# Hidden rows turned in 32 by 32 squares by VectorE and moved by DMA, for every other block of the first network

## What is computed

```python
# attention: state = alpha * state + k v^T; y = q . state      -> x (3072, 384)
expert_idx = np.argmax(xn @ en.T / tau, axis=1)                # 8 experts
for e in range(8):
    mask = expert_idx == e
    h = np.maximum(x[mask] @ w1[e], 0.0)                       # 384 -> 1024
    out[mask] = gate_w[mask, None] * (h @ w2[e])               # 1024 -> 384
h = out @ w_in                                                 # 384 -> 2048
y = np.maximum(0.01 * h, h) @ w_out                            # 2048 -> 384
```

## Time and profile before

| | us |
|---|---|
| median of 3 runs | 841.24 |
| lowest, highest | 840.91, 841.72 |
| the profiled execution's own time | 841.14 |
| its span, first to last instruction | 839.4 |
| PE busy | 826.0 |
| DVE busy | 418.4 |
| ACT busy | 340.4 |

### The profile page before, as it was taken

How to read it: one execution, slowest core, us unless ns; L and a number is a source line. 1 busy time by engine, 2 the same in 40 slices (tenths; PEclk the granted TensorE clock), 3 DMA queues, 4 the chain that set the end, 5 groups by cost and what they waited for, 6 DMA issues and landing times.

```text
span 839.4 us, 16998 instructions
## 1 busy us (share of the span) xinstructions
PE 826.0 (98%) x5491; PEld 742.7 (88%) x5492; DVE 418.4 (50%) x652; ACT 340.4 (41%) x643; POOL 197.4 (24%) x280
## 2 busy tenths in 40 slices
PE   7899999999999999999999999999999999999998
PEld 7788887999999999999999998998998998998997
DVE  7899986735544435445265433533533433443332
ACT  2545554634544425445254323323323333333223
POOL 6667623132233222332124003003003001000100
DMA  9988664435345332496002201201101000000001
GB/s 227 273 248 238 195 217 136 165 108 188 112 130 189 104 115 104 129 241 201 26 4 41 38 1 39 38 1 38 21 17 38 0 0 36 3 1 3 36 1 38
DMA packets 50454, 78.44 MB, mean 93 GB/s; under 512 B 22695, under 2 KB 39635, under 8 KB 50416
## 3 DMA queue, kind: packets, MB, share of 16 engines
q1 hardware_dynamic: 41232, 63.05, 26.1%
q0 software_dynamic: 5888, 14.85, 5.2%
q10 hardware_dynamic: 3296, 0.06, 0.2%
HBM read 63.69 MB, written 15.64 MB: 95 GB/s over the span
## 4 chain that ended last, share of the span: by engine, by line
PE 93%; DMA 3%; DVE 2%; POOL 1%; issue 1%; ACT 0%; SPq 0%; POOLq 0%; DVEq 0%
PE bank L1471 24%; PE bank L1506 24%; PE bank L1444 15%; PE bank L1424 15%; PE bank L1435 3%; DMA qkas<-qka 2%; PE bank L1266 2%; PE bank L1306 2%; PE bank L1283 2%; PE bank L1314 1%; PE bank L1400 1%; PE bank L1272 1%; PE bank L1326 1%; POOL kt L560 1%; DVE decay L874 0%
## 5 line engine op out<-in xcount | busy, mean ns | idle before, releaser
L1471 PE MATMUL bank<-yT,wts 128*128 128x512 f32 x864 | 217.0, 395 | 0.0
L1506 PE MATMUL bank<-wts,gs 128*128 128x384 f32 x1152 | 215.4, 335 | 0.4 <-ACT os L823 0.2
L1506 PEld LDWEIGHTS bank<-wts,gs 128*128 128x128 f32 x1152 | 202.1, 188 | 10.6 <-issue 1.6
L1471 PEld LDWEIGHTS bank<-yT,wts 128*128 128x128 f32 x864 | 160.7, 188 | 30.7
L1232 DVE TENSOR_TENSOR g<-bank,small 128x512 f32<-128x512 f32 x96 | 66.4, 692 | 174.1 <-ACT small L832 167.0
L1424 PE MATMUL bank<-wts,gxT 128*128 (+1 forms) x549 | 139.5, 398 | 0.2 <-issue 0.2
L1444 PE MATMUL bank<-wts,hT 128*128 x744 | 137.2, 339 | 0.0
L832 ACT ACTIVATE small<-bank 128x512 f32<-128x512 f32 x96 | 57.6, 600 | 187.3 <-PE bank L1471 165.7
L1444 PEld LDWEIGHTS bank<-wts,hT 128*128 128x128 f32 x744 | 128.5, 188 | 0.2
L1424 PEld LDWEIGHTS bank<-wts,gxT 128*128 128x128 f32 x549 | 100.2, 188 | 19.3 <-issue 0.8
L1234 DVE TENSOR_TENSOR gs<-g,gs 128x512 fp32r<-128x512 f32 x96 | 66.6, 693 | 67.0 <-ACT gs L835 61.5
(11 more groups left out here) (178 smaller groups left out, 728.9 us busy)
## 6 DMA issues: line engine op xcount, KB each, us to landing
raw<-w SPq DMA_DIRECT2D x14, 1536.0 KB, 7.2
qkas<-qka SPq DMA_DIRECT2D x20, 675.5 KB, 5.4
vs<-v SPq DMA_DIRECT2D x24, 192.0 KB, 3.8
x_rows<-xs SPq DMA_DIRECT2D x24, 192.0 KB, 3.9
yl<-y_rows SPq DMA_DIRECT2D x20, 192.0 KB
raw<-w_in SPq DMA_DIRECT2D x2, 1536.0 KB, 7.0
raw<-w_out SPq DMA_DIRECT2D x2, 1536.0 KB, 7.7
raw<-w SPq DMA_DIRECT2D x3, 512.0 KB, 5.5
```

The costliest lines, as they stand in the source:

```text
L1471: m = pe.matmul(gps[f % 2][:, :], wts[:, 0, w_part, n:n + P], yT[:, u, y_part, k], start=(k == 0 and (w_part, y_part) == (0, 0)), stop=(k ...
L1506: m = pe.matmul(ops[tt], gs[:, f % 4, g_part, tt * P:(tt + 1) * P], wts[:, 1, w_part, f * D:(f + 1) * D], start=(f == 0 and (g_part, w_par ...
```

## The change

For the even blocks 2, 4, ..., 28 (14 of the 31; `by_squares`), PE no longer turns the hidden rows. ACT writes ReLU's result to `hr`; DVE turns every 32 by 32 square of it within its 32 partitions (`turn_h` on DVE, one `transpose` of 128 by 512 for each half) into `hs`; SP issues 16 transfers of 32 partitions by 256 numbers (`move_h`, 1 KB rows) that bring the squares to their partitions in `hds`; ACT and DVE make `hT` from `hds`, in SBUF, in place of the banks. The rows of `w2` are put in another order ahead of the launch, so that the order of the hidden columns fits; ReLU of the other blocks writes its columns in that order too.

PE is two blocks ahead with `w1`: in the step of block `w` it does `hidden(w + 2)`. In the steps of odd blocks `turn_h(w)` stands between the halves as before, in those of even blocks nothing does. POOL gathers one block further ahead. Weights: the split of the next expert's `w1` is made two blocks ahead, in the step `w` where `w + 2` is an expert's first block, that of `w2` where `w` is. ACT makes the splits and then itself waits for DVE's part (`w1_lo`, `w2_lo`) and issues the load of the half after (`load_half`), 16 loads; SP keeps the first two. `wtab`'s flags are fewer, so DVE makes seven small vectors less before the first step. All weights come from one array in which a partition's 12 KB lie together (2 KB pieces; 4 KB and 1.5 KB before). Both first tiles of the second network's inner product stand before the last `contract`.

```diff
+        def by_squares(w, u):
+            return u == 0 and not (isinstance(w, int) and w in (0, WINDOWS - 1))
...
+        def load_half(eng, half, n):
+            eng.wait_ge(w_lo[half], n * 3)
+            at = slice(half * 3 * PC, (half + 1) * 3 * PC)
+            src = weights[n, half] if isinstance(n, int) else weights[ds(n, 1), half].rearrange("a p n -> (a p) n")
+            eng.dma_start(raw[:, at], src, max_dma_last_dim=2048).then_inc(raw_in[half], 16)
...
 SP
+            def move_h(w):
+                for j in range(QUADS):
+                    if j % 2 == 0:
+                        sp.wait_ge(h_turned, w - FIRST + j // 2 + 1)
+                    if j == 0 and not (isinstance(w, int) and w == FIRST):
+                        sp.wait_ge(ht_lo, w * 2 - 2)
+                    for i in range(QUADS):
+                        sp.dma_start(hds[j * SQ:(j + 1) * SQ, i * QF:(i + 1) * QF],
+                                     hs[i * SQ:(i + 1) * SQ, 0, j * QF:(j + 1) * QF]).then_inc(h_moved, 16)
...
 ACT
+            def h_round(w, u, half):
+                cols = slice(half * HALF, (half + 1) * HALF)
+                if not by_squares(w, u):
+                    act.wait_ge(ht_turned, turns_by_pe(w) + half + 1)
+                    act.activation(hT[:, 0, cols], htps[half][:, :], ACT.Copy).then_inc(ht_hi, 1)
+                    return
+                act.wait_ge(h_moved, w * 128)
+                act.wait_ge(ye_ready, w + 1)
+                act.activation(by_square(hT[:, 0, cols]), moved(half), ACT.Copy).then_inc(ht_hi, 1)
+            def first_weights(s, e):
+                wait_from(act, h_ready, s * 2)
+                split_hi(act, e, next_set(act, e), W1_PIECES)
+                load_half(act, 0, next_expert(act, e))
+            def second_weights(w, e):
+                act.wait_ge(ye_ready, w + 1)
+                split_hi(act, e, next_set(act, e), W2_PIECES)
+                load_half(act, 1, next_expert(act, e))
...
+            def step(w, u):
+                if isinstance(w, int) and w == 0:
+                    for half in range(2):
+                        relu(1, 1, half)
...
                 for half in range(2):
+                    h_round(w, u, half)
+                if isinstance(w, int) and w == 0:
+                    gx_round(2, 0)
+                    with act.If(act.snap(E - first) > 0):
+                        first_weights(0, 1)
+                if ahead(w, 2):
+                    for half in range(2):
+                        relu(w + 2, u, half)
+                if ahead(w, 3):
+                    gx_round(w + 3, 1 - u)
+                if ahead(w, 2):
+                    e, first = follower(act, w + 2)
+                    with act.If(first > 0):
+                        first_weights(w + 2, e)
+                e, first = follower(act, w)
+                with act.If(first > 0):
+                    second_weights(w, e)
...
 DVE
+            def turn_h(w, u):
                 for half in range(2):
+                    dve.wait_ge(relu_done, w * 2 + half + 1)
+                    dve.transpose(hs[:, u, half * HALF:(half + 1) * HALF].rearrange("p (n f) -> p n f", f=SQ),
+                                  hr[:, half].rearrange("p (n f) -> p n f", f=SQ)).then_inc(h_turned, 1)
...
+                for half in range(2):
+                    h_rest(w, u, half)
...
+                if ahead(w, 2) and by_squares(w + 2, u):
+                    turn_h(w + 2, u)
+                if ahead(w, 3):
+                    gx_rest(w + 3, 1 - u)
                 if isinstance(w, int) and w == 0:
                     place_slots()
...
 PE
+            def step(w, u):
+                if isinstance(w, int) and w == 0:
+                    block_hidden(1, 1)
+                if isinstance(w, int) and w == 0:
+                    turn_h(0, 0)
+                    turn_gx(2, 0)
+                if ahead(w, 2):
+                    block_hidden(w + 2, u, (lambda: turn_h(w, u)) if u == 1 else None)
+                elif not by_squares(w, u):
+                    turn_h(w, u)
+                if ahead(w, 3):
+                    turn_gx(w + 3, 1 - u)
+                if not ahead(w, 1):
+                    pe.wait_ge(w_lo[0], SET_IN * 3 + 3)
+                    pe.wait_ge(relu_done, WINDOWS * 2)
+                    for f in range(2):
+                        inner(0, 0, f)
...
                 contract(w, u, par)
```

More of the change, by code:

```diff
@@ L987, in _ @@
             W = WINDOWS
[L988 removed]
+            expert, first, code = (wflag[:, j, :] for j in range(3))
             start("side", dve.memset(cx, 0.0))
[L990 removed]
             start("side", dve.memset(first, 1.0))
```

276 lines of the change are left out of this document (132 added, 144 removed).

## The result

The changed kernel takes **846.6 us** in the median of 6 runs (843.48 to 847.44); the kernel before took 841.22 in its 6 (840.91 to 841.87). The ratio is 1.0054, 95% interval 1.0035 to 1.0074: slower by half a per cent, where 837.3 was forecast. The profiled execution took 847.34, its span is 845.3, 5.9 more than before's 839.4.

What follows compares the result with a forecast made beforehand. PE, busy 98% of the span, was taken to bound the kernel. From 841.14, -11.1 and -0.3, then +2.8, +1.4, +1.5 and +1.8 gave 837.2, or 837.3 on the median's scale; range 832.5 to 841.8.

Steps and rivals of the forecast that it cites:

- Removed transposes: PE's list in 14 even blocks: eight transposes of 0.79 us go from each, -11.1 us in all.
- The bound from above: Removed transposes: half 1's 0.08 longer time goes too if it came from the transposes ahead, -12.2 us.
- What replaces them in the loop: DVE's turning, SP's 16 moves and the rounding in even blocks: hidden by some 6 us of cover, cost 0.
- Weights on ACT: ACT's splits, wait for DVE and issue of loads: 0.9 us of cover left in the tightest odd step, cost 0.
- Step 0: `hidden(2)` stands right behind `turn_gx(2)`, whose result it reads: a PE gap of 2.8 us, bounds 1.4 and 4.
- step 29: `h(29)` is turned and contracted with nothing between: PE waits 1.5 us, bounds 1.1 and 1.6.
- The end: The third tile waits for `g` of the first, no longer covered by the second tile: +1.8 us, bounds 0 and 2.1.
- Earlier tables: Seven DVE vectors go before the first step, so `hidden(1)` may start at once: -0.3 us, bounds -0.4 and 0.
- Step 1: PE waits for `hT(1)` behind ACT's and DVE's splits and tables: a gap of 1.4 us, bounds 0 and 3.
- The rival of the slower clock: PE at half clock for another 5.06 us behind the gap in step 0: 2.5 us more, 839.8; chance 0.09.
- The rival of lost cover: Splits' steps or DVE's longer list overrun their cover in the loop, 0.3 us a block over 14: 841.4; chance 0.07.
- The other rivals: Moves set the pace, 910, chance 0.07; the gaps are not there, 831.8, 0.10; half 1 slower, 846, 0.03.

Runs made afterwards that it cites:

- the fills: The changed kernel with 12 fill matmuls of PE in the wait of step 0 and 11 in that of step 1: 842.21 us.
- the run with late loads: The changed kernel with ACT issuing each load of weights one step later, between the two ReLUs of the next block: 843.19 us.
- Four orders: Changed kernel, 846.6; its start and end in the old order, 843.38; ACT and DVE reordered in steps 0 and 1, 845.25; all four edits, PE turning block 2, 837.03.
- the last of the four orders: The changed kernel with one table read, other start order, both end edits, and PE turning block 2 too (`FIRST` 4): 837.03 us.

## Why the prediction was wrong

*Removed transposes, -11.1.* Mis-sized, in the good direction: -13.3. An even block lost 0.90 and the odd one behind it 0.05. The bound from above, -12.2, was too tight. I took the 0.79 between two starts as the whole price, but half 1 behind the transposes also ran 0.08 longer (2.16 against 2.08), and the rest, 0.03 and 0.05, I had nowhere.

*What replaces them in the loop, 0.* Right in the end, on wrong numbers, so with luck. An issue took 0.591 us, not 0.43, so 16 took 9.4 to 9.6; still under the 0.96 at which I had it decide. Sixteen fixed costs of 2 us one behind the other would be 32 us a pair, and the pair took 18.15, so they do overlap; the Trainium skill (DMA: Bandwidth & Descriptors, Anatomy of one DMA) gives those 2 us for transfers that GpSimd issues, and these are SP's. But the cover was not 6 us: beside a load of weights the rows landed so late that ACT waited 4.91 for them, and `hT` was ready 0.85 before PE wanted it (253.56 + 1.29 against 255.70). In eight of the even blocks ACT waited so for moved rows, 5.1 us on average, and in blocks 10 to 18 between 0.5 and 1.2 was left. I had put both on separate queues and taken them as apart.

*Weights on ACT, 0.* **This is the step that failed.** It put the cover behind a split in an odd step at 0.9 and the cost at nothing; it cost 5.5. For the splits of `w1` I had the time at which ACT is free right, 11.9 into the step (214.93 is 12.0 in). I then let ACT round at once. It did not: 1.38 us of register work lie between, and rounding, rest and PE's start took 1.72 where I had 1.28. For the splits of `w2` ACT was free only at 12.9 (235.25), since both reads stood ahead of the split, with 0.54 behind. Either way cover 0.9 became a wait of 0.8 to 1.0 and its restart, four times: +4.8; block 3 the same way, +0.7. The sum had no term for register work on ACT at all.

How much of it is the read that the change added (ACT and DVE read twice a step where they read once)? From `contract(2)` to `contract(30)` the kernel gains 2.3 us when ACT reads once and 2.5 when DVE does too. So the added read is nearly half of the 5.5. The rest stays with one read: four waits of 0.42 to 0.48 with their restarts, in steps where ACT also waits for DVE's last piece and issues. Its parts were not told apart. By the Trainium skill (Advanced Engine Details and Errata, Control Flow Timing) a branch with a compare takes about 0.1 us; the trace's rows of ACT's branch behind a read have 0.034 to 0.050, a small part of a read's 0.68, of which the load takes 0.285.

*Step 0, +2.8*: 2.88, and *step 29, +1.5*: 1.27 and the restart, 1.5. *The end, +1.8*: 1.62, 1.9 with the restart. *Earlier tables, -0.3*: -0.24, and `hidden(1)` did follow at once. *Step 1, +1.4*: 2.48, within its bounds of 0 to 3. ACT's chain there had the same hole, and DVE, too, idled 2.05 us behind `place_slots`.

*The rival of the slower clock* (0.09, +2.5) came true as well, behind both gaps: +3.2. I had argued that PE was busy for long before and that the gap was shorter than the first one, and by the rule I had kept the price for the longest gap only; it fell behind the shorter one, 2.48, as well. By the Trainium skill (TensorE: Matmul & The Clock Gate, The HAM clock gate) idleness brings the array to half rate; this trace agrees, with 0.50 and 0.51 behind waits of 2.48 and 2.88, and the fills show that work in the gap prevents it. Which wait does it and which doesn't, no run here settles: the run with late loads kept 1.00 behind 2.77 and 2.19.

*The rival of lost cover* (0.07, 841.4) named the place and priced it at 4.2 where it cost 5.5. It and the clock came together, 8.7 on top of the forecast's gaps, which no single rival held. The other rivals fell: 16 issues did not set the pace, the gaps were there, and half 1 behind half 0 was no slower.

*Left open.* How to free the start. Four orders gave PE's waits in steps 0 to 2 of 2.9 and 2.5, 2.0 and 2.7, 1.3 and 4.6, 1.0 and 2.9 (with one turn more). In the changed kernel the trace shows what is last before `contract(1)`: DVE's split of `w2`, which starts 2.05 us of register work behind `place_slots` and holds ACT's rounding of block 1.

```profile
163.79 3.50 DVE L415 TENSOR_TENSOR wts<-raw,wts 128x1024 f32 x3 [2.05 <-issue]
...
167.91 1.09 ACT L815 ACTIVATE hT<-bank 128x512 fp32r<-128x512 f32 x2 [5.49 <-DVE wts L415]
```

In the last of the four orders the same split, now behind DVE's logits, and then ACT's exponential are what block 2 waits for. No run moved the logits and the exponential, so what that would gain is not shown.

Against the sum of 837.2, the profiled 847.34 is 10.1 more: lost cover 5.5, the clock 3.2, the attention 1.55, step 1 1.3, other gaps 0.5, less the turns' 2.2, and 0.3 outside the span (2.04 in place of 1.74).

## What to carry to other kernels

Count an engine's register work, reads and branches as a term of its chain: here one table read more in each step cost 2.3 to 2.5 us and the next one 5.5, while the transfers that the change was about cost nothing in the loop, and the view of engines' busy time doesn't show it; the idle time ended by "issue" does. Work taken from the engine that sets the pace also takes cover from the others: of 13 us of removed turns 4.1 went into waits. Where a wait like those here (1.8 us and up) is opened on PE, add the clock's price to it, and fill it if it can't be closed. Price a wait as its idle time and the restart.

## What the runs showed of the hardware

- SP's issue of a 32 KB transfer from SBUF to SBUF takes 0.591 us (median of 224, 0.507 to 1.561), the 48 KB ones of the earlier trace rows 0.43.
- A third read of the table on ACT, with its branch, cost 5.5 us in 28 blocks.
- In the profiled executions of the changed kernel and its variants PE waited 26 times for 1.81 to 4.56 us in steps 0 to 2, and behind 17 of these waits its clock was at 0.50. It fell behind one of 1.81 and stayed at 1.00 behind one of 2.92. A fall cost 1.6 to 1.7 us in the changed kernel; behind waits of 4.01 and 4.56 the 24 matmuls took 7.04 and 6.89 where 4.4 is usual.
- With the same code executions lie 6.4 us apart, at mean clocks of 1.0 to 0.992.
- DVE turns the 32 by 32 squares of 128 by 512 numbers in 0.705 us (median of 28).
